# A recurrent-attention and mixture-of-experts kernel: the fourth head pair's outputs placed in the free rows of the others, the dense layer's input split straight from PSUM, tiles started before the turn ends

## The reference

```python
for t in range(S):
    cur = np.einsum('bhd,bhe->bhde', u[None] * kt, vt)
    y[:, :, t] = np.einsum('bhd,bhde->bhe', rt, state + cur)
    state = wt[:, :, :, None] * state + np.einsum('bhd,bhe->bhde', kt, vt)
```

## Time and profile before

| | |
|---|---|
| median of 3 runs | 538.54 us (535.93 to 540.98) |
| profiled execution | 538.73 us, of which the span from first to last instruction is 537.0 us |
| PE busy | 471.9 us (88% of the span) |
| DVE busy | 322.5 us (60%) |
| ACT busy | 216.7 us (40%) |
| mean granted clock of PE | 0.937 of full speed |

### The profile page before, as it was taken

One profiled execution on the slowest core, in us unless ns is written; L12 is line 12 of the kernel. 1 busy time (PEld: TensorE's weight loads), 2 busy tenths in 40 slices (PEclk: granted clock), 3 DMA queues, 4 the chain that ended last, 5 costly groups with the idle time before them and its releaser, 6 DMA issues.

```text
span 537.0 us, 15350 instructions
## 1 busy us (share of the span) xinstructions
PE 471.9 (88%) x6230; PEld 442.9 (82%) x6231; DVE 322.5 (60%) x824; ACT 216.7 (40%) x458; POOL 46.3 (9%) x63
## 2 busy tenths in 40 slices
PE   3757999899998999799989999993398599999994
PEld 3656898789997899799978999993398488989994
DVE  5986748675567635873676354545254199869520
ACT  2421345224322333242412344344154299868520
POOL 5000000000010001000100001102001022222201
PEclk9995999979997999999989999997599799999998
DMA  8708971900060005100100010000837089786001
GB/s 282 270 23 300 364 272 35 380 10 4 11 205 5 3 1 169 51 2 2 37 28 1 2 31 31 30 1 11 284 110 250 26 306 338 281 293 232 26 1 40
DMA packets 38023, 63.76 MB, mean 119 GB/s; under 512 B 4316, under 2 KB 24590, under 8 KB 37952
## 3 DMA queue, kind: packets, MB, share of 16 engines
q1 hardware_dynamic: 35648, 58.27, 31.4%
q0 software_dynamic: 2304, 4.47, 2.3%
HBM read 48.80 MB, written 14.19 MB: 117 GB/s over the span
## 4 chain that ended last, share of the span: by engine, by line
PE 78%; DVE 9%; issue 5%; DMA 3%; ACT 2%; SPq 2%; POOL 0%; DVEq 0%; POOLq 0%; ACTq 0%
PE bank L540 20%; PE bank L528 19%; PE bank L674 10%; PE bank L641 6%; PE pair L468 6%; PE pair L434 4%; PE pair L641 2%; PE pair L653 2%; PE pair L506 2%; PE pair L490 2%; PE pair L674 2%; PE pair L497 2%; PE pair L555 1%; DVE AD L931 1%; DVE KRW L911 1%
## 5 line engine op out<-in xcount | busy, mean ns | idle before, releaser
L528 PE MATMUL bank<-XH,W 128*128 128x256 f32 x576 | 129.6, 302 | 9.5 <-DVE XL L957 8.7
L528 PEld LDWEIGHTS bank<-XH,W 128*128 128x128 f32 x576 | 100.2, 199 | 11.7 <-DVE XL L957 8.8
L540 PE MATMUL bank<-W,GH 128*128 128x384 f32 x384 | 103.7, 352 | 0.5 <-ACT X L715 0.5
L715 ACT ACTIVATE GH<-GG 128x256 fp32r<-128x256 f32 x96 | 40.1, 417 | 140.4 <-DVE GG L962 140.2
L528 PE MATMUL bank<-XL,W 128*128 128x256 f32 x288 | 83.9, 291 | 0.0
L468 PE MATMUL pair<-KRW 48*64 48x32 f32 (+1 forms) x2304 | 54.0, 238 | 21.8 <-DVE KRW L913 14.5
L468 PEld LDWEIGHTS pair<-KRW 48*64 48x64 f32 (+1 forms) x2304 | 45.9, 154 | 32.2 <-DVE KRW L913 17.8
L1041 DVE TENSOR_TENSOR W<-stage,W 128x768 fp32r<-128x768 f32 x64 | 58.4, 953 | 22.7 <-ACT W L715 21.9
L540 PEld LDWEIGHTS bank<-W,GH 128*128 128x128 f32 x384 | 66.7, 192 | 2.0 <-ACT X L715 0.7
L715 ACT ACTIVATE W<-stage 128x768 fp32r<-128x768 f32 (+1 forms) x72 | 62.6, 918 | 12.3 <-DMA stage<-in_moe_w_in 10.8
L540 PE MATMUL bank<-W,GL 128*128 128x384 f32 x192 | 65.7, 342 | 0.0
(11 more groups left out here) (129 smaller groups left out, 671.7 us busy)
## 6 DMA issues: line engine op xcount, KB each, us to landing
stage<-in_moe_w SPq DMA_DIRECT2D x32, 768.0 KB, 5.4
KRW<-in_krw SPq DMA_DIRECT2D x12, 512.0 KB, 6.7
slots<-X SPq DMA_DIRECT2D x1, 4632.0 KB, 23.2
XG<-slots SPq DMA_DIRECT2D x24, 193.0 KB
KRW<-in_krw SPq DMA_DIRECT2D x12, 256.0 KB, 7.0
stage<-in_moe_w_in SPq DMA_DIRECT2D x4, 768.0 KB, 6.4
stage<-in_moe_w_out SPq DMA_DIRECT2D x4, 768.0 KB
VV<-in_v SPq DMA_DIRECT2D x12, 256.0 KB, 9.4
```

What stands on the lines that cost most here:

```text
L528: last = nc.tensor.matmul(bank[4 + f % 2][:, 0:2 * P], win[wa][:, c, f * P:(f + 1) * P], xa[:, c, :], start=n == 0, stop=n == 3 * KM - 1)
L540: last = nc.tensor.matmul(bank[6 + m][:, 0:DM], ga[f % G4][:, cols], wout[wa][:, f, :], start=f == 0 and n == 0, stop=f == NF - 1 and n == 2)
L715: return nc.scalar.activation(dst, src, ACT.Copy)
```

## The change

1. The fourth head pair (q = 3) no longer has output columns of its own. Its 48 output rows per head are cut in three parts of 16, and each is written by PE into the 16 free partitions beside the outputs of pair 0, 1 or 2 (L510 and L535 of the new kernel, stationary operands of 32 columns whose first 16 are zeros from the padded values). A tile's outputs so fill all 128 partitions in three blocks, which is the layout of the dense layer's input; `w_in`'s rows are permuted to match when the inputs are sent. The state for q = 3 is 96 columns wide instead of 48; SA, SM, SD and a half of IN go from 192 to 240 columns.
2. OT, X3 and the ten transfers per turn are gone. ACT reads XH's half of 384 columns per tile from the PSUM pair, DVE reads the same bank for XL. XH and XL are doubled, so that a group's input can be made while the last is in use.
3. Slots run over turn borders. `due` looks in the tables of this turn and the next. From group 2 on tile t = 0 starts at slot 13 of the turn before (levels 0, 1, 2 there) and tile t = 1 at slot 4. The last three `project` of a turn stand in slots 0 to 2 of the next. The gate moves to slots 7 to 11, its small results to banks 0 and 1.
4. Level 0 of a tile waits for `xl_ready` in place of `ot_ready`. Chunks 4 to 6 of the weights and the tiles of group 2 no longer have a repack ahead of them in SP's queue; chunk splits move to slots 3, 5, 7, 9 (ACT) and 1, 5, 7, 9, 11 (DVE) of turn 1.

```diff
-    NPIECE = sum(-(-(h + 1) * D // P) - h * D // P for h in range(H))
     G4 = 4
     NSTEP = 7
-    AT_SLOT = ((0, 1, 2, 4, 5, 6, 7, 8, 10), (0, 1, 2, 4, 5, 6, 7, 8, 11))
...
-    STATE_SLOT = (9, 10)
-    UK_SLOT = (11, 12)
-    HIGH_SLOT = ((0, 1, 2, 3), (6, 8, 10, 12))
-    LOW_SLOT = ((6, 7, 12, 13), (7, 9, 11, 13))
-    GATE_SLOT = 11
-    LAG = 1
+    QF = HP - 1
+    DR = DP - D
+    VW = DP + DR
+    SW = QF * D + QF * 2 * DR
+    SQ = SW // D
+    FIRST = ((0, 1, 2, 3, 4, 5, 6, 7, 9), (0, 1, 2, 3, 4, 5, 6, 7, 10))
+    SECOND = ((-1, 1, 2, 3, 4, 5, 6, 7, 9), (4, 5, 6, 7, 8, 9, 10, 11, 13))
+    LATER = ((-3, -2, -1, 0, 1, 2, 3, 4, 6), (4, 5, 6, 7, 8, 9, 10, 11, 13))
+    UK_SLOT = (-6, 2)
+    HIGH_SLOT = (0, 1, 2, 3, 19, 21, 23, 25)
+    LOW_SLOT = (6, 7, 12, 17, 21, 23, 25, 27)
+    GATE_SLOT = 7
+    PL = 3
...
-        KRW = [[sb(f"KRW{t}{n}", [P, off[-1] + H], on=p1) for n in range(2)] for t in range(2)]
-        VV = [[sb(f"VV{t}{n}", [P, H, DP], on=p1) for n in range(2)] for t in range(2)]
+        KRW = [[sb(f"KRW{t}{n}", [P, off[-1] + 2 * SQ], on=p1) for n in range(2)] for t in range(2)]
+        VV = [[sb(f"VV{t}{n}", [P, 2, QF, VW], on=p1) for n in range(2)] for t in range(2)]
...
-        OT = sb("OT", [P, HP, 2, P], on=p1)
-        X3 = sb("X3", [P, KM, 2 * P], on=p1)
...
+        SA = sb("SA", [P, SW], on=p1)
+        SM = sb("SM", [P, SW], on=p1)
+        SD = sb("SD", [P, SW], on=p1)
+        IN = [sb(f"IN{t}", [P, 2, SW], on=p1) for t in range(2)]
+        XH = [sb(f"XH{n}", [P, KM, 2 * P], F32R, on=p1) for n in range(2)]
+        XL = [sb(f"XL{n}", [P, KM, 2 * P], F32R, on=p1) for n in range(2)]
...
+        def table(n, t):
+            return (FIRST, SECOND, LATER)[min(n, 2)][t]
+
+        def due(i, t, s):
+
+            for n in (i, i + 1):
+                x = s - NF * (n - i)
+                if n < NG and x in table(n, t):
+                    return n, table(n, t).index(x)
+            return None, None
+
+        def due_from_last(i, t, s, d):
+
+            return i if i < NG and s - d == table(i, t)[-1] else None
...
+        def x_of(x, i, t):
+
+            return x[i % 2][:, :, t * P:(t + 1) * P].rearrange("p k (h n) -> p h k n", h=2)
+
+        def made_x(t):
+            return pair[t][:, :, 0:QF * C].rearrange("p h (k n) -> p h k n", k=QF)
...
-            def repack(i):
-                for t in range(2):
-                    sp.wait_ge(ot_ready[t], i + 1)
-                need(sp, xl_ready, i)
-                need(sp, xh_ready, i)
-                for h, d, c, n in pieces:
-                    src = OT[DP * (h % 2) + d:DP * (h % 2) + d + n, h // 2, :, :].rearrange("p t n -> p (t n)")
-                    sp.dma_start(X3[c % P:c % P + n, c // P, :], src).then_inc(ld_x3, 16)
...
-            repack(0)
             for n in range(CH, NW0):
+                if n == NW0 - 1:
+                    for t in range(2):
+                        load_tile(2, t)
+                        load_v(2, t)
...
-            for i in range(1, NG):
-                for t in range(2) if i + 1 < NG else ():
-                    load_tile(i + 1, t)
-                    load_v(i + 1, t)
-                repack(i)
-                for c in range(CH) if i == 1 else ():
-                    sp.wait_ge(wl_ready, NW0 + c - CH + 1)
-                    sp.dma_start(staged(c, expert_chunk(0, 0, c)[2]), expert_chunk(0, 0, c)[0]).then_inc(ld_w[c], 16)
+            for c in range(CH):
+                sp.wait_ge(wl_ready, NW0 + c - CH + 1)
+                sp.dma_start(staged(c, expert_chunk(0, 0, c)[2]), expert_chunk(0, 0, c)[0]).then_inc(ld_w[c], 16)
+            for i in range(3, NG):
+                for t in range(2):
+                    load_tile(i, t)
+                    load_v(i, t)
...
-                    need(pe, ot_ready[t], i)
-                    need(pe, end_ready, 2 * (i - 1) + t + 1)
-                    if t == 1:
+                    need(pe, xl_ready[t], i)
+                    if t == 0:
...
-                    for q in range(HP):
+                    for q in range(QF):
                         for a in range(2):
-                            nc.tensor.matmul(pair[t][DP * a:DP * (a + 1), h, q * C:(q + 1) * C], vv[rows, 2 * q + a, :],
+                            nc.tensor.matmul(pair[t][DP * a:DP * (a + 1), h, q * C:(q + 1) * C], vv[rows, a, q, 0:DP],
                                              AD[t][rows, HP * a + q, :], start=q == 0, stop=False, skip_group_check=True)
+                    for q in range(QF):
+                        for a in range(2):
+                            nc.tensor.matmul(pair[t][DP * (a + 1) - 2 * DR:DP * (a + 1), h, q * C:(q + 1) * C],
+                                             vv[rows, a, q, D:VW], AD[t][rows, HP * a + QF, :],
+                                             start=False, stop=False, skip_group_check=True)
                 for h in range(2):
                     rows = slice(C * h, C * (h + 1))
                     for q in range(HP):
                         for a in range(2):
-                            c = 2 * P + q * DP
-                            last = nc.tensor.matmul(pair[t][DP * a:DP * (a + 1), h, c:c + D],
-                                                    KN[t][rows, q * P + DP * a:q * P + DP * (a + 1)], vv[rows, 2 * q + a, 0:D],
+                            c = 2 * P + q * D
+                            moved, w = (vv[rows, a, q, 0:D], D) if q < QF else (vv[rows, a, :, D:VW], SW - QF * D)
+                            last = nc.tensor.matmul(pair[t][DP * a:DP * (a + 1), h, c:c + w],
+                                                    KN[t][rows, q * P + DP * a:q * P + DP * (a + 1)], moved,
                                                     start=False, stop=q == HP - 1, skip_group_check=True)
                 last.then_inc(inc_done[t], 1)
...
-                        last = nc.tensor.matmul(pair[t][DP * a:DP * a + D, h, q * C:(q + 1) * C], x[rows, q, :],
-                                                KRW[t][i % 2][rows, c:c + C], start=False, stop=q == HP - 1,
-                                                skip_group_check=True)
+                        reads = KRW[t][i % 2][rows, c:c + C]
+                        if q < QF:
+                            nc.tensor.matmul(pair[t][DP * a:DP * a + D, h, q * C:(q + 1) * C], x[rows, q * D:(q + 1) * D],
+                                             reads, start=False, stop=False, skip_group_check=True)
+                        else:
+                            for n in range(QF):
+                                c = QF * D + 2 * DR * n
+                                last = nc.tensor.matmul(pair[t][DP * (a + 1) - 2 * DR:DP * (a + 1), h, n * C:(n + 1) * C],
+                                                        x[rows, c:c + 2 * DR], reads, start=False, stop=n == QF - 1,
+                                                        skip_group_check=True)
...
+                    if mlp:
+                        hidden(i - 1, s)
                     if attn:
                         attention(i, 0, s)
-                    if mlp and s >= lag + 3:
-                        if s == lag + 3:
-                            need(pe, x2_ready, 2 * (i - 1))
-                        project(i - 1, s - lag - 3)
+                    if mlp:
+                        g, f = before_slot(i - 1, s, PL)
+                        if f == 0:
+                            need(pe, x2_ready, 2 * g)
+                        if g is not None:
+                            project(g, f)
...
-                copy(IN[t][:, :, :, :], pair[t][:, :, 2 * P:2 * P + HP * DP].rearrange("p h (q e) -> p h q e", q=HP)[:, :, :, 0:D]
-                     ).then_inc(inc_ready[t], 1)
-
-            def outputs_back(i, t):
+                copy(IN[t][:, :, :], pair[t][:, :, 2 * P:2 * P + SW]).then_inc(inc_ready[t], 1)
+
+            def x_high(i, t):
                 act.wait_ge(mid_read, 2 * i + t + 1)
-                need(act, ld_x3, 16 * NPIECE * i)
-                copy(OT[:, :, t, :].rearrange("p q (h n) -> p h q n", h=2),
-                     pair[t][:, :, 0:2 * P].rearrange("p h (q n) -> p h q n", q=HP)).then_inc(ot_ready[t], 1)
-
-            def x_high(i, mlp):
-                act.wait_ge(ld_x3, 16 * NPIECE * (i + 1))
-                if mlp:
-                    act.wait_ge(h_done, NF * i)
-                copy(XH[:, :, :], X3[:, :, :]).then_inc(xh_ready, 1)
+                need(act, h_done, NF * (i - 1))
+                copy(x_of(XH, i, t), made_x(t)).then_inc(xh_ready[t], 1)
...
-            def x_low(i):
-                dve.wait_ge(xh_ready, i + 1)
-                tt(XL[:, :, :], X3[:, :, :], XH[:, :, :].bitcast(F32), ALU.subtract).then_inc(xl_ready, 1)
+                tt(SA[:, :], SD[:, :], IN[t][:, 1], ALU.add).then_inc(end_ready, 1)
+
+            def x_low(i, t):
+                dve.wait_ge(xh_ready[t], i + 1)
```

(15 more changed lines are left out.)

171 lines of the change are left out of this document (76 added, 95 removed).

## The result

| | before | changed |
|---|---|---|
| median of the runs | 537.23 us (535.74 to 540.98, 4 runs) | 552.37 us (552.27 to 558.42, 4 runs) |
| profiled execution, its span | 538.73, 537.0 us | 552.36, 550.6 us |
| first `hidden` starts | 44.27 us | 43.26 us |
| last `project` ends | 364.03 us | 376.24 us |
| `outputs` block of a tile | 1.46 us | 2.85 us |

The change makes the kernel slower: the ratio is 1.030, interval [1.021, 1.039]. 531.2 was forecast, and 552.4 lies above the range (521 to 541).

The account below looks back on a forecast made before the run. PE was taken to bound turns 1 to 5, through its waits, clock and added work. From 538.73 us, -8.5 - 5.8 + 1.1 - 9.6 - 0.8 - 5.75 + 14.0 + 3.2 + 4.6 = -7.55 gave 531.2 us, range 521 to 541.

Parts of the forecast that it names:

- 2, 3, 4, 5 and 7 together: Turns 1 to 5: clock, waits and, as 3, level 0 of group 1's tile 1 now standing in turn 1, +1.1 us.
- Step 6: PE, ten tiles: columns of `outputs` +0.57, of `state_outputs` +0.51, third term seven width changes 0.32; +14.0 us in all.
- Step 1: First border: without the repack the first `hidden` starts at 35.8 us instead of 44.27, -8.5 us.
- Step 2: Behind the first border: PE's work from 44.3 to 55.9 us runs at 2.4 instead of 1.2 GHz, -5.8 us.
- Steps 4 and 5: 4: border waits of turns 2 to 5 -9.6 us, turn 1's waits -0.8; 5: clock of turns 2, 3, 5 -5.75 us.
- Step 7: New PE waits for DVE: behind slot 13 and at slots 5 and 6 +3.2 us, in turn 1 +4.6 us.
- D: Rival: placement costs more than borders give, by slow narrow matmuls and full 0.09 us shape changes; 548.8 us, chance 0.07.
- B: Rival: the clock keeps falling, once in each of turns 1 to 4 at 1.9 us; 538.9 us, chance 0.15.
- C: Rival: the second x_low comes late, each border waits 2 us, four times; 539 us, chance 0.05.
- A: Rival: narrow matmuls are nearly free, the 1.40 us surcharge per tile is halved; 523 us, chance 0.17.
- a turn 4 above 58 us: Sign that the forecast is wrong; turns 2 to 4 were expected at about 56 to 57 us each.

Follow-up runs that it names:

- e9: Nothing placed, the fourth pair left out of the dense input, plus level 0 a slot earlier and one chunk split later, against the changed kernel: 524.32 us, ratio 0.972 to before.
- e6: The changed kernel with all placed products, in `outputs` and `state_outputs`, at 64 stationary columns, so no width change is left: 544.43 us, ratio 1.010 to the kernel before.
- e1: The changed kernel with the placed products of `outputs` padded to 64 columns, `state_outputs` still narrow: 540.18 us, ratio 1.002 to the kernel before.
- e2: The changed kernel's same matmuls reordered, two width changes each in `outputs` and `state_outputs` instead of four and three: 545.17 us, ratio 1.010 to the kernel before.
- e8: The changed kernel with wide and narrow pairs of `outputs` in turns, twelve width changes per tile instead of four: 569.77 us, ratio 1.060 to the kernel before.
- e5: The changed kernel with every tile's steps back inside their own turn, direct read and placement kept: 576.09 us, ratio 1.062 to the kernel before.
- e3: The changed kernel with nothing placed: fourth pair in its own columns, its part left out of the dense input: 530.21 us, ratio 0.983 to the kernel before.
- e11: e10 with the placement as twelve 64 x 64 products, two halves side by side, instead of six of full height: 529.59 us, ratio 0.985 to the kernel before.
- e10: Full computation with e9's slots: fourth pair in its own columns, copied by ACT, placed once by six full-height selection matmuls: 538.74 us, ratio 1.002 to the kernel before.
- e4: The changed kernel with nine full-size matmuls at its start and one more per slot of turn 0: 555.33 us, ratio 1.021 to the kernel before.

## Why the prediction was wrong

Measured against the span, as the prediction's sum was made (537.0 to 550.6, +13.6), in place of -7.55:

| step | forecast | measured |
|---|---|---|
| 1, first border | -8.5 | -1.0 |
| 6, added PE work on ten tiles | +14.0 | +24.8 |
| 2, 3, 4, 5 and 7 together | -13.05 | -11.6 |
| behind the last `project` | 0 | +1.4 |

The third row is what is left of the stretch from the first `hidden` to the last `project` (319.76 us before, 332.98 now) when 24.8 is taken off. It is not the worth of these steps by themselves: in e9, where nothing is placed, the same stretch is only 7.1 us shorter than before.

**Step 6 failed in its third term.** The columns were right: with them alone the two blocks are 2.00 and 1.67 us (e6), 1.18 more than before, and 1.08 was forecast for them. The width changes were put at 7 x 0.045, "between 0 and 0.09", and they cost 4.97 - 3.67 = 1.30 us per tile, 0.19 each. The bound was wrong, not the choice in it. It came from a change of height behind a large matmul, and there the next block, L468, only starts 0.09 us later; here a change also parts two groups that ran side by side, and that overlap was not in the row that I took. The sentence of the Trainium skill ("TensorEngine Tiling (Array Packing)", Key Properties: a change of tiling mode drains the engine) names the mechanism; e1, e2 and e8 agree with it, and show twice the price that I gave it. Step 6 also said that the rule would make 534.4, which it doesn't. In turn 0 the step counted one half of `state_outputs` in the way of the first `hidden`; the trace has three.

**Step 1 failed by the clock, and by a block that was to be hidden.** What was added in front of the first `hidden` was priced at full clock. In the kernel before the records of turn 0 get short at 28.9 us, and I took that for granted. With the narrow bursts they do so at 46 us, and with the wide ones of e6 at 32.3. Of the 5.4 us that turn 0 loses by it 0.8 are in the kernel before too, so 4.6 of the missing 7.5 us are the clock's. Next, level 0 of group 1 was to hide behind the rounding. It doesn't: it stands between the last `state_outputs` and the first `hidden`, which makes 1.9 us in e9 (0.80 of waiting for XL and 1.13 for the level) and 1.9 in the changed kernel (the level alone, at half clock), where 1.15 was forecast. The rest is step 6 again: the placed work of turn 0 would be 4.4 us at full clock (2 x 1.39 + 3 x 0.545) and not 1.8; 0.4 us of waits and of a later start in the kernel before go the other way. Why the clock rises late isn't shown. All kernels here with narrow bursts in turn 0 have long records until 44 us or later, those without until 29 to 33, but e5, with the same turn 0 as the changed kernel, has them until 77.9.

**Step 2** was given back in part: the gap at 39 us is gone, but from the first `hidden` on PE is at half clock for 2.7 us, and behind the wait of 1.59 us at 52.55 for 3.3, 6.0 us in place of 11.6. In e9 the fall behind the wait of 1.44 us in turn 1 took nearly all of it back. **Steps 4 and 5**: no wait for `update` above 0.24 us at slots 0 to 2 and no fall of the clock in turns 2 to 5, as forecast. Step 4 took turn 4's 3.0 us of waits for all four turns; the earlier trace rows has 2.5, 2.6, 3.0 and 2.3. And e5 loses these waits as well, so that the `project` moved into slots 0 to 2 is enough for it there. **Step 7** was right behind slot 13 and too high in turn 1 (0.38 and 1.59 for 1.8 and 1.9; its own terms for slot 2, 5.2 us on DVE against 3.0 on PE, make 2.2). The run behind the last `project` was forecast unchanged; what makes the 1.4 us more there stays open.

**The rivals.** D, at 0.07, had the right sign and the nearest time, 548.8. Of its two mechanisms the slow narrow matmul is wrong (e2) and the dearer change right. Alone it stays 1.08 us per tile above item 6, short of the 1.27 from which the kernel would be slower by 1%; with turn 0 at half clock it is. So its time was near partly by luck: turn 0 is no part of it. B is wrong for turns 2 to 4 of the changed kernel, where one fall in turn 1 is all there is, but right for a faster one (e6, e3). C is wrong: no border waits for the input. A is wrong: the narrow matmuls were not nearly free. The prediction's own sign of being wrong, a turn 4 above 58 us, is there (59.4).

## What to carry to other kernels

Count the changes between stationary shapes as instructions of their own, each with a price of 0.1 to 0.3 us here, and pad an operand with zeros to the width of its neighbours before making it narrow: 48 columns of zeros cost PE nothing that its blocks show, and taking out the four changes of `outputs` gave 12 us (e1). Place a result once, after it is summed, and in the shape of the blocks beside it (e11, not e10). Where a step is sped up, look first at what waits behind it: e6 was shorter than e1 by 0.45 us per tile and by 2.9 us at the first border, and lost more than that to longer waits for DVE and the clock behind them, until two slots were moved. And before a difference is put down to waits, compare the durations of one known matmul in both kernels: e5's 22 us looked like its slots and were the clock.

## What the runs showed of the hardware

- Between 64 and 32 stationary columns, at a height of 64 rows: 0, 2, 4 and 12 changes give blocks of 2.00, 2.22, 2.85 and 3.91 us. Twelve narrow matmuls in one burst take 0.61 us, twelve wide ones 0.67. Between 48 and 32 columns, 3 and 2 changes give 2.12 and 1.86 us with the same matmuls.
- The clock column of a kernel's first stretch can't be trusted: it says 1.00 in the changed kernel from 27 to 46 us and in e5 to 77.9, while every matmul takes the time that it has at 1.2 GHz (L558 0.41 against 0.28). With earlier full-size matmuls in e4 the same stretch is shown as 0.50. The durations tell it.
- A fall of the clock does not last a fixed time: some 3 us behind two of the 1.40 us waits of e6, 34 us in e5, where PE was busy all the while with blocks of 64 rows between full-size ones. The wait before it does not settle it either: 0.93 and 1.07 us were never followed by one here, 1.40 in two of four turns (e6), 1.58 in one of three (e3), and gaps of 0.28 to 0.41 us in a row of such blocks were in e5 at 174 us and in e10, but not in e5 at 245 us.
- Six full-height fp32 products of 128 x 128 with 64 moved columns take 1.25 to 1.48 us (e10), twelve of 64 x 64 in two halves side by side 0.64 to 0.84 us in all (e11).
